# Up to 32 leftover rows of an expert as a small unit on four column groups in plain fp32; the first expert's padding set behind its first 512 rows

## The reference

```python
logits = x @ w_gate + modality_bias[modality_id]
e_idx = np.argmax(logits, axis=1)
...
for e in range(E):                       # E = 8
    mask = e_idx == e
    h = np.maximum(x[mask] @ w1[e], 0.0)            # 512 -> 1024
    out[mask] = gate_w[mask, None] * (h @ w2[e])    # 1024 -> 512
```

## Time and profile before

| | before |
|---|---|
| median of 3 runs | 899.33 us (898.9 to 899.98) |
| the profiled execution: its time, its span | 899.0 us, 897.0 us |
| PE busy | 878.1 us (98% of the span) |
| DVE, ACT, POOL busy | 634.5, 385.8, 179.8 us |
| granted TensorE clock | 0.997 of full speed |
| last instruction of a matrix product | 886.3 us |

### The profile page before, as it was taken

The page is one execution under the profiler, slowest core; times in us unless marked ns, Lnnn a source line. Parts: engine busy times, 40 slices in busy tenths (PEclk is TensorE's granted clock), DMA queues, the critical chain, the costliest instruction groups (busy, mean ns, idle before and its releaser), DMA issues.

```text
span 897.0 us, 22411 instructions
## 1 busy us (share of the span) xinstructions
PE 878.1 (98%) x8014; PEld 823.0 (92%) x8014; DVE 634.5 (71%) x1491; ACT 385.8 (43%) x936; POOL 179.8 (20%) x289
## 2 busy tenths in 40 slices
PE   7999999999999999999999999999999999999995
PEld 6787999999999999999999999999899999999994
DVE  6776776875876876776785773268677777777765
ACT  3556434343342443443343332251455555555553
POOL 2451112222222231231332221002100000000000
PEclk9999999999999999999999999999999999999998
DMA  8734623123133122222222212044641117111111
GB/s 227 207 119 160 218 70 95 49 81 110 33 92 97 57 81 82 66 78 80 72 84 60 84 37 84 9 180 154 197 117 47 47 47 232 48 48 47 47 47 29
DMA packets 95736, 83.39 MB, mean 93 GB/s; under 512 B 51487, under 2 KB 75551, under 8 KB 95648
## 3 DMA queue, kind: packets, MB, share of 16 engines
q1 hardware_dynamic: 91120, 68.55, 26.2%
q0 software_dynamic: 4240, 13.66, 4.1%
q10 hardware_dynamic: 288, 0.00, 0.0%
HBM read 56.70 MB, written 25.74 MB: 92 GB/s over the span
## 4 chain that ended last, share of the span: by engine, by line
PE 94%; DVE 2%; ACT 1%; issue 1%; DMA 1%; DVEq 0%; ACTq 0%; POOL 0%; SPq 0%; POOLq 0%
PE acc_a L336 7%; PE acc_b L336 6%; PE acc_b L337 6%; PE acc_b L338 6%; PE acc_a L337 6%; PE acc_a L338 6%; PE misc L330 4%; PE misc L331 4%; PE misc L332 4%; PE s_even L970 3%; PE acc_a L330 3%; PE acc_b L330 3%; PE attn L331 2%; PE attn L332 2%; PE attn L330 2%; PE acc_a L331 2%
## 5 line engine op out<-in xcount | busy, mean ns | idle before, releaser
L836 POOL TENSOR_TENSOR probs<-scores,row_inv 128x256 f32<-128x256 f32 x96 | 66.9, 717 | 278.4 <-DVE row_inv L1914 278.4
L1389 ACT ACTIVATE ew<-raw_e 128x1024 fp32r (+1 forms) x100 | 101.2, 1050 | 12.2 <-issue 11.1
L336 PE MATMUL acc_a<-xT_w,w 128*128 128x384 f32 x256 | 89.4, 349 | 0.0
L336 PE MATMUL acc_b<-xT_w,w 128*128 128x384 f32 x256 | 87.9, 343 | 0.0
L337 PE MATMUL acc_a<-xT_w,w 128*128 128x384 f32 x256 | 86.5, 338 | 0.0
L337 PE MATMUL acc_b<-xT_w,w 128*128 128x384 f32 x256 | 86.5, 338 | 0.0
L338 PE MATMUL acc_b<-xT_w,w 128*128 128x384 f32 x256 | 86.5, 338 | 0.0
L338 PE MATMUL acc_a<-xT_w,w 128*128 128x384 f32 x256 | 86.5, 338 | 0.0
L1415 ACT ACTIVATE scores<-scores,neg_max 128x136 f32<-128x136 f32 x192 | 75.9, 398 | 19.5 <-DVE neg_max L1904 19.5
L912 POOL DMA_INDIRECT out<-row_out,ids_i x25 | 26.9, 1076 | 239.0 <-DVE row_out L2083 213.9
L1389 ACT ACTIVATE uT_w<-ab 128x384 fp32r<-128x384 f32 x64 | 33.3, 520 | 93.3 <-DVE ab L1966 93.3
(11 more groups left out here) (377 smaller groups left out, 2963.2 us busy)
## 6 DMA issues: line engine op xcount, KB each, us to landing
raw_e<-in_moe_w SPq DMA_DIRECT2D x24, 512.0 KB, 8.6
raw<-in_moe_w SPq DMA_DIRECT2D x16, 512.0 KB, 5.9
x_in<-routed SPq DMA_DIRECT2D x108, 64.0 KB, 1.9
v_nat<-in_v SPq DMA_DIRECT2D x24, 256.0 KB, 3.1
x_mid<-x_out SPq DMA_DIRECT2D x24, 256.0 KB, 2.0
x_in<-x_mid SPq DMA_DIRECT2D x24, 256.0 KB, 2.8
q_nat<-in_q SPq DMA_DIRECT2D x80, 64.0 KB, 2.3
k_nat<-in_k SPq DMA_DIRECT2D x80, 64.0 KB, 2.0
```

What stands on the lines that cost most here:

```text
L336: pe.matmul(o, w_hi, x_hi, start=start, stop=False, skip_group_check=True)
L836: pool.tensor_tensor(probs[:, at, side * HALF:(side + 1) * HALF], scores[:, at, side, SINKS:], row_inv[:, at].unsqueeze(2).broadcast_to([P ...
L1389: return act.activation(o, i, ACT.Copy)
```

## The change

1. **The small unit.** A remainder of an expert becomes a pair if it has more than 32 rows, and otherwise a unit `few` of 32 rows. PE then uses the 32 rows of x as the stationary operand on each of four groups of 32 columns: group g makes hidden columns 256g to 256g + 255, later output columns 128g to 128g + 127. The products are plain fp32, so ACT copies the expert's weights unsplit into `few_w`, and no low parts are made. The results of the four groups lie on 4 x 32 partitions; two transposes turn the hidden rows. SP loads gate and token number four times, once for each group of partitions (`few_gates`), DVE works out the row numbers for an output seen as rows of 128 (`few_ids`), and POOL writes it.
2. **Bounds of the loops.** PAIRED becomes 11 and MOST_PAIRS 19 (UNITS stays 19).
3. **The padding.** The first expert's padding is set at its end or behind its first 512 rows, whichever is later. The waits for the rows of unit 1 fall away on SP and POOL, and SP issues its four right after `ends_known`, ahead of the wait for the last rows (`row_sent`) and of the rows of unit 1. The wait for all eight moves behind `gates_done`, to the rows of unit 2.
4. **The tables on DVE.** `second` gives the start of a pair's second tile (its own formula for a unit `few`), `spread_no` is new, and `rows_i` of both tiles are made in a new order.
5. The semaphore `zeroed` is merged into `consts` (same operations, same order).

```diff
+    FEW = 32
+    SPREAD = P // FEW
+    PAIRED = (N - E * FEW) // EXPERT_ROWS
+    MOST_PAIRS = E + (N - E * (FEW + 1)) // EXPERT_ROWS + 1
+    UNITS = E + (N - E) // EXPERT_ROWS
...
@@ sync
+            sp.wait_ge(ends_known, 1)
+            for e in range(0, E, 2):
+                end = sp.value_load(ends_i[0:1, e:e + 1], min_val=0, max_val=PAD_ROW - P)
+                sp.dma_start(routed[bass.ds(end, P), :], padding[:, :]).then_inc(pad_sent, 16)
 
             for r in row_sent:
                 sp.wait_ge(r, TILES // GT * 16)
...
-            sp.wait_ge(ends_known, 1)
-            for tile in range(2):
-                sp.wait_ge(slot_in[tile], slots_in(1))
-            for e in range(0, E, 2):
-                end = sp.value_load(ends_i[0:1, e:e + 1], min_val=0, max_val=PAD_ROW - P)
-                sp.dma_start(routed[bass.ds(end, P), :], padding[:, :]).then_inc(pad_sent, 16)
-            sp.wait_ge(pad_sent, E // 2 * 16)
-            sp.wait_ge(pad_sent_odd, E // 2 * 16)
...
-            def single(u):
+            def few(u):
                 next_expert(u)
-                sp.wait_ge(gates_done, u + 2)
+                sp.wait_ge(y_done[0], u)
+                sp.sem_inc(own_wait[1], 1)
+                at = sp.value_load(rows_i[0:1, 0, bass.ds(u, 1)], min_val=0, max_val=PAD_ROW)
+                for mine in spread:
+                    sp.dma_start(few_gates[mine, :], routed[bass.ds(at, FEW), DM:ROW]).then_inc(few_in, 16)
                 load_tile(u + 2, 0)
 
             sp.wait_ge(known, ROWS)
             sp.wait_ge(gates_done, 2)
+            sp.wait_ge(pad_sent, E // 2 * 16)
+            sp.wait_ge(pad_sent_odd, E // 2 * 16)
@@ tensor
+            def few(u):
+                pe.wait_ge(X_full[0], u + 1)
+                pe.wait_ge(h_lo, 8 * u + H_BEFORE)
+                for c in range(KD):
+                    pe.wait_ge(e1_hi, splits_before(u) + KD + c + 1)
+                    for g, mine in enumerate(spread):
+                        mm = pe.matmul(s_even[mine, 0:2 * P], x_turned[:, c, 0:FEW], few_w1[c][:, g * 2 * P:(g + 1) * 2 * P],
+                                       start=c == 0, stop=c == KD - 1, skip_group_check=True)
+                mm.then_inc(h_full, 4)
+                pe.wait_ge(h_hi, 8 * u + 8)
+                for part in range(2):
+                    mm = pe.transpose(s_odd[:, part * P:(part + 1) * P], few_h[:, part * P:(part + 1) * P], ident[:, :])
+                mm.then_inc(h_full, 4)
+                pe.wait_ge(h_lo, 8 * u + H_BEFORE + 8)
+                pe.wait_ge(y_done[0], u)
+                for c in range(KF):
+                    pe.wait_ge(e2_hi, splits_before(u) + c // 2 + 1)
+                    for g, mine in enumerate(spread):
+                        at = c % 2 * P + c // 2 * FEW
+                        mm = pe.matmul(attn[mine, 0:P], few_hT[:, at:at + FEW], few_w2[c // 2][:, c % 2 * DM + g * P:c % 2 * DM + (g + 1) * P],
+                                       start=c == 0, stop=c == KF - 1, skip_group_check=True)
+                mm.then_inc(y_full[0], 1)
@@ scalar
+            def few(u):
+                need, buf = weights_of(u)
+                act.wait_ge(h_full, 8 * u)
+                for c in range(KD):
+                    act.wait_ge(expert_in[c], need * 2 + 16)
+                    act.wait_ge(e1_lo, n_pairs * KD + (c + 1))
+                    copy(few_w1[c], raw_chunk(buf, 0, c)).then_inc(e1_hi, 1)
+                act.wait_ge(y_full[0], u)
+                for c in range(KD):
+                    if c == 2:
+                        act.wait_ge(h_full, 8 * u + 4)
+                        act.activation(few_h, s_even[:, 0:2 * P], ACT.Relu).then_inc(h_hi, 8)
+                    act.wait_ge(expert_in[KD + c], need * 2 + 16)
+                    copy(few_w2[c], raw_chunk(buf, 1, c)).then_inc(e2_hi, 1)
@@ vector
+            def few(u, j):
+                ve.wait_ge(h_full, 8 * u + 8)
+                ve.wait_ge(y_full[0], u)
+                ve.tensor_copy(few_hT, s_odd[:, 0:2 * P]).then_inc(h_lo, 8)
+                ve.wait_ge(few_in, j * (SPREAD * 16) + SPREAD * 16)
+                ve.wait_ge(y_sent[0], 16 * u)
+                ve.tensor_scalar(few_ids[:, :], few_gates[:, 1:2], float(SPREAD), spread_no[:, 0:1], ALU.mult, ALU.add)
+                ve.wait_ge(slot_in[0], slots_in(u + 1))
+                ve.transpose(x_turned[:, :, 0:P].rearrange("p c (f j) -> p c f j", f=4),
+                             x_in[:, 0, 0:DM].rearrange("p (f n c) -> p c f n", f=4, c=KD)).then_inc(X_full[0], 1)
+                ve.wait_ge(y_full[0], u + 1)
+                ve.tensor_scalar(row_out[:, 0, 0:P], y_banks[0][:, 0:P], few_gates[:, 0:1], None, ALU.mult).then_inc(y_done[0], 1)
...
+            op(ve.tensor_reduce(f[3], slot_b[:, :, :], AX.X, ALU.add))
+            op(ve.tensor_scalar(rows_i[:, 0, :], f[0], float(PAD_ROW), None, ALU.add))
             turn_x(1, 0)
             turn_x(1, 1)
```

More of the change, by code:

```diff
@@ L132, in build @@
             ew = sb("ew", [P, 4, KD * F], F32R, staged)
+        with ExitStack() as staged:
+            sb("before_few", [P, 4, KD * F], F32, staged)
+            few_w = sb("few_w", [P, 2, KD * F], F32, staged)
         sb("early_home", [P, 8, KD * F])
@@ L140, in build @@
             x_turned = sb("x_turned", [P, KD, EXPERT_ROWS], F32, last)
+            few_rows = sb("few_rows", [P, 2, 2 * P], F32, last)
         raw8 = sb("raw8", [P, 8, WIDE * 2])
@@ L386, in x_of @@
             return x_turned[:, :, tile * P:(tile + 1) * P]
+        few_w1, few_w2 = ([few_w[:, part, c * CH:(c + 1) * CH] for c in range(KD)] for part in range(2))
+        few_h, few_hT = few_rows[:, 0, :], few_rows[:, 1, :]
+        spread = [slice(FEW * g, FEW * g + FEW) for g in range(SPREAD)]
+        out_spread = out.rearrange("n (g d) -> (n g) d", g=SPREAD)
         BH = B * H
@@ L898, in _ @@
             pool.wait_ge(ends_known, 1)
-            for tile in range(2):
-                pool.wait_ge(slot_in[tile], slots_in(1))
             for e in range(1, E, 2):
@@ L918, in pair @@
                     send_out(u, tile)
+            def few(u):
+                pool.wait_ge(y_done[0], u + 1)
+                pool.sem_inc(own_wait[2], 1)
+                pool.indirect_dma_start(out_spread, bass.IndirectOffsetOnAxis(few_ids[:, 0:1], 0),
+                                        row_out[:, 0, 0:P], None, bounds_check=SPREAD * N - 1, oob_is_err=False)\
+                    .then_inc(y_sent[0], 16)
             pair(0)
@@ L1365, in pair @@
                 unit_y(u, 1)
-            def single(u):
-                for k in range(KF):
-                    unit_h(u, 1, k)
-                unit_y(u, 0)
+            def few(u):
[20 more added lines that the diff above has]
+                mm.then_inc(y_full[0], 1)
             pair(1)
@@ L1689, in _, with pair @@
             n_singles = act.value_load(units_i[0:1, 1:2], min_val=0, max_val=E)
-            def unit_y(u):
-                act.wait_ge(gates_done, u + 1)
-                act.wait_ge(y_full[0], u + 1)
-                act.wait_ge(y_sent[0], 16 * u)
-                act.activation(ids_i[:, 0:1], gates_r[:, 0, 1:2], ACT.Copy)
-                act.activation(row_out[:, 0, 0:DM], y_banks[0][:, :], ACT.Copy, scale=gates_r[:, 0, 0:1]).then_inc(y_done[0], 1)
-                act.wait_ge(y_done[0], u + 1)
-                copy(gates_r[:, 0:1, :], x_in[:, 0:1, DM:ROW]).then_inc(gates_done, 1)
-            def unit(u, tiles):
+            def pair(u):
                 need, buf = weights_of(u)
                 for k in range(KF):
-                    unit_h(u, tiles, k)
+                    unit_h(u, 2, k)
                     if k == 0:
                         act.wait_ge(y_full[0], u)
-                        act.wait_ge(y_full[1], u if tiles == 2 else n_pairs)
+                        act.wait_ge(y_full[1], u)
                     if k < KD:
@@ L2258, in _ @@
             first_no = ctl[:, 14, 0:1]
-            units_of, some, order, region_2, start, place_k, end, base, place_p, prev_start, mark = (job[:, j, :] for j in range(11))
+            units_of, some, order, region_2, start, place_k, end, base, place_p, prev_start, mark, second = (job[:, j, :] for j in range(12))
             pairs_of, singles_of = units_of[:, 0:E], units_of[:, E:JOBS]
@@ L2334, in _ @@
             op(ve.tensor_tensor(f[0], f[0], f[1], ALU.add))
-            op(ve.tensor_tensor(slot_b[:, :, :], slot_a[:, :, :], inner(place_k, by_unit), ALU.mult))
+            op(ve.tensor_tensor(slot_b[:, :, :], slot_a[:, :, :], inner(second, by_unit), ALU.mult))
+            done()
+            op(ve.tensor_reduce(f[3], slot_b[:, :, :], AX.X, ALU.add))
+            op(ve.tensor_scalar(rows_i[:, 0, :], f[0], float(PAD_ROW), None, ALU.add))
             turn_x(1, 0)
```

83 lines of the change are left out of this document (36 added, 47 removed).

## The result

The changed kernel takes 903.52 us (median of 5 runs, 902.97 to 904.04), the kernel before in the same call 899.39 us (898.9 to 899.98). The ratio is 1.0045, 95% interval [1.003, 1.006]: slower by 4.1 us, beyond the range of 898.6 to 901.8 and beyond the 0.2% (1.8 us) that a measurement can tell. The profiled execution of after took 903.78 us, with a span of 902.1 (899.0 and 897.0 before).

A forecast was written before the change was run, and what follows sets the result against it. PE was taken to bound the kernel (busy 878 of 897 us), with SP ending it. The hole's -0.87 and the end's +1.3 made +0.4 on the median of 899.33, about 899.8 us; range 898.6 to 901.8.

The forecast's parts named there:

- cost 0, bounds 0 and 1: At unit 1: the early padding costs PE 0 us, at most 1, since DVE's later start just fits the room.
- I count 0.8 us of delay, so the second tile lands near 618.7: At unit 1: early padding delays the rows by 0.8 us, second tile at 618.7 instead of 617.9.
- the padding stands in the way: Rival at unit 1: padding writes delay its rows, some 2.5 us, giving 902.3 us; chance 0.14.
- The hole ahead of unit 2: PE's idle time ahead of unit 2 goes with the earlier padding: -0.87 us.
- near 625: SP's rows of unit 2 start near 625.5 instead of 629.3, waiting for the second copy of the gates alone.
- The small unit on PE: At the end: PE reaches the small unit at about 871.8, and its second part ends near 878.8.
- the prediction's estimate for groups side by side: Small unit on PE: four column groups together take 1.75 us for each part, and 0.3 to drain each.
- the 7.0 us for them: Small unit on PE: bound of 7.0 us for each part if the groups ran one after another.
- The gates chain on SP: At the end: SP's skipped passes and four gate loads release it at 889.1 instead of 887.83, +1.3 us.
- a rival of its own, for +1.05: Rival at the end: seven third-loop passes on SP at 0.65 us, +1.05, so 900.8; within the forecast's 0.62.
- Three more passes cost 1.95 us: SP's second loop: seven skipped passes instead of four, about 0.65 us each, bring it to its wait 1.95 us later.
- The saving doesn't reach the end: At the end: PE's shorter products gain nothing, as SP is busy; the opposite rival had 890.0 us, chance 0.05.

The follow-up runs named there:

- e4: The changed kernel, but POOL's four paddings wait for the rows of unit 1 as before, SP's stay early: 900.54 us, ratio 1.0017.
- g1: The changed kernel, but SP's four paddings are issued after the rows of unit 1 have landed, POOL's stay early: 899.50 us, ratio 1.0008.
- f4: The kernel before with loops that skip no passes on all engines, nothing else: 894.33 us, ratio 0.9959.
- f3: f1 with loops that skip no passes on all five engines: 892.04 us, ratio 0.9929.
- e3: The changed kernel with MOST_PAIRS 16 instead of 19, so four skipped passes of the second loop instead of seven: 900.96 us, ratio 1.0023.
- e1: The changed kernel with the padding issued in the old place and order: 900.96 us, ratio 1.0023.
- f1: The changed kernel with SP's paddings directly behind the rows of unit 1, POOL's once these have landed: 899.39 us, ratio 1.0012.
- f2: f1 with DVE's transposition of the next rows ahead of its wait for the small gates: 897.11 us, ratio 0.9985.
- e2: The kernel before with the change's early padding alone; units, tables and loops as before: 902.68 us, ratio 1.0038.
- g2: f3 and f2 together: late paddings, no skipped passes, early transposition on DVE; 891.14 us, ratio 0.9912.
- g3: g2 with one transfer for the small gates instead of four: 890.75 us, ratio 0.9913.

## Why the prediction was wrong

- **The step that failed: "cost 0, bounds 0 and 1" for the early padding.** It rested on "I count 0.8 us of delay, so the second tile lands near 618.7". It landed at 621.8, and PE lost 2.94 us. The count took the order of issue for a protection ("the last rows are issued at 607.9, ahead of most paddings"). The order was about as it says: of the eight only SP's first, at 606.5, went ahead of the last row transfer at 607.0. But the sixteen DMA engines were busy for 0.99 of the time from 607 to 613 and for all of it up to 619, and the transfers issued first were slowed as well. So the delay comes twice in series: the row transfer lands 1.7 us later than before, SP starts later by that, and then the rows wait among POOL's paddings (e4, g1). The count also had only the second tile in view; the first, complete at 620.8 instead of 615.4, would have held DVE by itself.
- **The term that was missing: the clock.** Behind the idle time the granted clock was 1.2 GHz for 3.4 us, and PE lost 1.5 us by it. The rival "the padding stands in the way" was right in mechanism, with a chance of 0.14, but its 2.5 us were 3.1 for the wait and 1.5 for the clock, 4.6 in all.
- **The hole ahead of unit 2: right, -0.87 of idle time** (-1.12 by the starts of the products), though a slow issue of SP had a part in it that the prediction doesn't name (f4). Rows of unit 2 "near 625" was wrong: 628.3, as the whole of unit 1 had moved.
- **The small unit on PE: right.** Without the 3.22 us PE reached it at 871.8 (871.8 predicted), the first part took 1.93 (2.05), and the second ended at 880.4 (878.8), since it ran at 1.2 GHz (3.47 us; at full clock 1.95, f3). The Trainium skill (TensorEngine Tiling (Array Packing), Overview) gives up to 4 times for dimensions of 32 or less. The 1.93 us agree with the prediction's estimate for groups side by side; no run here has the groups one by one, and the 7.0 us for them stay an estimate.
- **The gates chain on SP: right in mechanism, +1.96 instead of +1.3.** Less 3.22, SP came to its wait at 883.55 (883.8), to the last issue at 885.8 (886.2), and was released at 888.6 (889.1): +0.8 so far. Then its five loads took 0.45 us longer, and the seven passes of the third loop 0.65 us each and not the 0.50 of the earlier trace rows, +1.1; some 0.4 came back behind them. That was a rival of its own, for +1.05.
- **Three more passes cost 1.95 us, as predicted:** e3 took just this off again between the first skipped pass and the wait. By the Trainium skill (Advanced Engine Details and Errata, Control Flow Timing), with about 108 ns for a compare-and-branch, six of them would be 0.65 us, an estimate; the trace does not agree.
- **"The saving doesn't reach the end": right.** In f3, the first kernel in which it could, the tail is 2.2 us shorter than with the single and no skips (f4).

The sum again, with what was measured: -1.12 for the hole (-0.87 predicted), +1.96 for the end (+1.3), +3.10 for the wait at unit 1 (0), +1.48 for the clock, -0.22 for the start-up and -0.02 of rest (none of the three in the sum) = +5.2 of span.

## What to carry to other kernels

A transfer that is moved ahead in time must be held against every transfer that is on its way with it, on any queue and whichever was issued first, and against whoever waits for those; writes that nobody reads soon belong behind the reads that the busiest engine waits for. A unit that saves products at the end of a kernel gives nothing if the queue that feeds it is in order and busy: shorten first what stands ahead of its loads, here skipped loop passes. Compare tails from a common point, since the middle of a run moves by as much as the edit is worth.

## What the hardware showed

- Granted clock: behind PE's idle time of 1.01, 1.56 and 1.90 us it stayed at 2.4 GHz; behind 2.94 us it was 1.2 GHz for 3.4 us, behind 3.37 us for 6.8 us. So 0.4 us more of idle time went with 3.4 us more at the low clock. But the length of the idle time does not decide alone: in the small unit PE stands idle for 1.87, 0.56 and 2.2 us in after, e1, f1, e4, f2 and g1 alike, and its second part took 3.47, 3.48, 2.58, 1.95, 1.95 and 1.95 us. PE's timeline of f2, which answers to the 3.47 us of after:

```profile
875.88 1.95 PE L1412 MATMUL attn<-few_w,few_rows 128*32 128x128 f32 x64 [2.22 <-DVE few_rows L2478]
```

- A direct load of 64 KB that lands 1.8 us after its issue took 5.0 to 5.6 us among eight writes of 257 KB, with the DMA engines busy for all of the time. An indirect row transfer took 3.3 us before, 6.0 in after, 6.9 in e4 and 7.3 in e2 among SP's writes, but 3.5 in g1 with POOL's writes alone, issued right behind it.
- Now and then one issue takes up to 1.8 us instead of 0.32 on SP or 0.98 on POOL, at various places in each kernel (631.3 in before, 877.7 in e3; one of the first four for unit 1 in after, e1, e2, e3, f2, f3, g1, g2 and g3, 0.91 to 1.50 us). It cost 1.1 us in e3 and had a part in the hole ahead of unit 2. What it waits for stays open.
- The same loop of seven skipped passes on SP takes 0.50 us a pass in the kernel before and 0.65 in after; why was not tried.
- POOL's drain is over 4.4 us after its start, or 4.4 us after the end of an indirect transfer that is still being issued when it starts (5.49 us in f3): 4.4 us that no engine covers once POOL is last.
